# Strassen's scheme for the products with w1 and w2, with g and w34 kept in DRAM between two phases

## What is computed

```python
k_p = k.reshape(B, H, Sp, 8, D).mean(axis=3)            # 72 pooled keys per head, v_p likewise
scores = scale * q @ k_p.T;  attn = exp(scores - max);  attn /= attn.sum() + 1e-9
x = attn @ v_p                                          # 4608 x 512
a, b = x @ w1, x @ w2                                   # w1, w2: 512 x 1024
x = ((a * b) @ w3) @ w_out                              # w3: 1024 x 1024, w_out: 1024 x 512
logits = x @ w_gate + modality_bias[modality_id];  e = argmax(logits);  g = softmax(logits)[e]
out = g * (relu(x @ moe2_w1[e]) @ moe2_w2[e])           # one expert per token
```

## Time and profile before

| | |
|---|---|
| median of 3 runs | 1207.93 us |
| profiled execution | 1200.84 us |
| its span, first to last instruction | 1198.8 us |
| mean granted TensorE clock | 0.997 |

### The profile page before, as it was taken

The page is one execution under the profiler, slowest core; times in us unless marked ns, Lnnn a source line. Parts: engine busy times, 40 slices in busy tenths (PEclk is TensorE's granted clock), DMA queues, the critical chain, the costliest instruction groups (busy, mean ns, idle before and its releaser), DMA issues.

```text
span 1198.8 us, 26051 instructions
## 1 busy us (share of the span) xinstructions
PE 1181.9 (99%) x10830; PEld 1043.9 (87%) x10831; DVE 523.4 (44%) x1158; ACT 265.0 (22%) x517; POOL 210.9 (18%) x245
## 2 busy tenths in 40 slices
PE   9999999999999999999999999999999999999996
PEld 7888888989889788897888989898999999899895
DVE  1657556475563754746414144622222243222221
ACT  1233222222222222222212124111111141111110
POOL 2234222022220222102000001121221112121111
PEclk9999999999999999999999999999999999999998
DMA  9552132230231312303000005151111101111111
GB/s 350 175 190 85 70 104 85 72 119 36 87 102 52 103 63 86 111 30 94 10 28 1 36 1 202 34 183 58 44 61 35 44 26 54 44 45 51 35 50 39
DMA packets 43295, 92.76 MB, mean 77 GB/s; under 512 B 9411, under 2 KB 18755, under 8 KB 42180
## 3 DMA queue, kind: packets, MB, share of 16 engines
q1 hardware_dynamic: 34356, 66.68, 16.7%
q0 software_dynamic: 6400, 20.50, 5.3%
q10 hardware_dynamic: 2448, 4.26, 1.0%
HBM read 70.93 MB, written 21.01 MB: 77 GB/s over the span
## 4 chain that ended last, share of the span: by engine, by line
PE 96%; DVE 2%; DMA 1%; issue 0%; ACT 0%; POOLq 0%; DVEq 0%
PE ab L709 17%; PE ab L710 17%; PE ab L711 17%; PE rt L709 6%; PE x2p L709 6%; PE x2p L711 6%; PE x2p L710 6%; PE rt L710 6%; PE rt L711 6%; PE sct L780 3%; PE ab L802 2%; PE ab L728 2%; PE sct L878 1%; PE x2p L728 1%; DMA w3b<-in_moe_w 1%; PE rt L728 1%
## 5 line engine op out<-in xcount | busy, mean ns | idle before, releaser
L709 PE MATMUL ab<-xth,e1h 128*128 128x256 f32 x608 | 169.5, 279 | 1.5 <-issue 1.5
L710 PE MATMUL ab<-xtl,e1h 128*128 128x256 f32 x608 | 170.5, 280 | 0.0
L711 PE MATMUL ab<-xth,e1l 128*128 128x256 f32 x608 | 169.3, 278 | 0.0
L1152 ACT ACTIVATE hth<-ab 128x512 fp32r<-128x512 f32 x76 | 45.5, 598 | 341.8 <-PE ab L711 341.8
L1595 DVE SCALAR_TENSOR_TENSOR htl<-ab,hth 128x512 fp32r<-128x512 f32 x76 | 52.3, 691 | 157.1 <-ACT hth L1152 157.0
L709 PEld LDWEIGHTS ab<-xth,e1h 128*128 128x128 f32 x608 | 114.1, 188 | 2.6 <-issue 1.9
L709 PE MATMUL ab<-xh,w1h 128*128 128x512 f32 x288 | 116.1, 403 | 0.0
L1245 DVE TENSOR_TENSOR ac<-ab,ac 128x512 f32<-128x512 f32 x72 | 49.8, 691 | 149.6 <-PE ab L711 91.8
L710 PEld LDWEIGHTS ab<-xtl,e1h 128*128 128x128 f32 x608 | 114.4, 188 | 0.7
L711 PEld LDWEIGHTS ab<-xth,e1l 128*128 128x128 f32 x608 | 114.2, 188 | 0.0
L710 PE MATMUL ab<-xl,w1h 128*128 128x512 f32 x288 | 112.9, 392 | 0.0
(11 more groups left out here) (200 smaller groups left out, 2394.8 us busy)
## 6 DMA issues: line engine op xcount, KB each, us to landing
kv<-in_v SPq DMA_DIRECT2D x24, 512.0 KB, 4.8
qt<-in_q SPq DMA_DIRECT2D x8, 1280.0 KB, 6.3
kv<-in_k SPq DMA_DIRECT2D x16, 576.0 KB, 7.9
x_rows<-xr SPq DMA_DIRECT2D x36, 256.0 KB, 3.3
stage<-in_moe_w SPq DMA_DIRECT2D x8, 1024.0 KB, 9.7
vp<-v_rows SPq DMA_DIRECT2D x32, 192.0 KB, 3.7
w3b<-in_moe_w ACTq DMA_DIRECT2D x16, 256.0 KB, 5.5
wo_t<-in_w_out_t SPq DMA_DIRECT2D x4, 512.0 KB, 8.7
```

What stands on the lines that cost most here:

```text
L709: pe.matmul(outp, lh, rh, start=first, stop=False)
L710: pe.matmul(outp, lh, rl, start=False, stop=False)
L711: return pe.matmul(outp, ll, rh, start=False, stop=last)
L1152: act.activation(hth[:, 2 * n:2 * n + 2, :].rearrange("p f n -> p (f n)"), ab[n // 2][:, n % 2, :], ACT.Relu).then_inc(hth_ready, 1)
```

## The change

- **Order.** All nine stages of products with w1 and w2 run first, then all 36 groups of products with w34. g goes to DRAM (`g_rows`) and comes back group by group through five pairs of buffers (`RING`), and is split into hi and lo when it comes back. w34 goes to DRAM (`w34_rows`) from the start and comes back before the second phase. The leftover tokens of each batch go to DRAM too (`left_x`).
- **Strassen (Winograd's form).** For each of 4 positions in a stage, x (512 tokens by 512) and the weights are cut in 2 x 2 blocks; seven block products replace eight. The seven sums or blocks of x (`xf`: `x_sum`) and of w1, w2 (`wr`: `w_sums`) are formed and split ahead of them (`hi_x`, `lo_x`, `hi_w`, `lo_w`). Each `product` has 2 x 2 x 3 matmuls of 128x256 (w1 into one half of a bank, w2 into the other), and three banks are used in turn. DVE adds each product's bank onto partial sums (`kb`) in SBUF (seven additions of 128x512 per position, and one copy on ACT), then multiplies a by b (`g_first`, `g_rest`).
- **Softmax.** `soft_max` takes only the maxima and scales them; `exp_p` is eight activations of 128x72 per round, one for each head, straight from PSUM with the maximum as bias and the sum as a second output; `norm`, eight activations on ACT, replaces the multiplication on DVE. A new round of scores now waits for `exp_done` instead of `sub_done`. ACT issues the loads of q and the stores of g and w34.
- **Routing** tables run in the second phase, in banks that are free there.
- The expert stage is the same but for its places in SBUF.

The core of the diff ("..." for what is left out):

```diff
+BLOCKS = 7
+POS = FC // 2
+HT = MAIN // 2
+RING = 5
+TABLE_AT = {4: (0, 1), 6: (2, 3)}
...
+            def product(b, i, n):
+                at, fs = POS * b + i, slice(P * i, P * (i + 1))
+                bank = product_bank(at, n)
+                if i == 0:
+                    pe.wait_ge(xl_ready, BLOCKS * b + n + 1)
+                if n == 3:
+                    pe.wait_ge(x_copied, at + 1)
+                elif n > 3:
+                    pe.wait_ge(c_taken, 7 * at + n - 3)
+                elif at:
+                    pe.wait_ge(c_taken, 7 * at + n - 2)
...
+                for m in range(2):
+                    if b == 0 and i == 0:
+                        pe.wait_ge(wl_ready, BLOCKS * m + n + 1)
+                    for c in range(2):
+                        mm = split(bank[:, HT * m:HT * (m + 1)], wh[:, m, n, c, fs], wl[:, m, n, c, fs],
+                                   xh[:, n, c, :], xl[:, n, c, :], m == 0 and c == 0, m == 1 and c == 1)
+                mm.then_inc(prod_done[n], 1)
+
+            def position(b, i):
+                if i == 0 and b == 0:
+                    score(1, 0)
+                if i == 1 and b + 1 < B:
+                    score(b + 1, 2)
+                if i == 2 and b + 1 < B:
+                    score(b + 1, 4)
+                if i == 3 and b + 2 < B:
+                    score(b + 2, 0)
+                for n in range(BLOCKS):
+                    product(b, i, n)
+                    if i == 0 and n == 3 and b + 1 < B:
+                        score(b + 1, 1)
+                    if i == 1 and n == 3 and b + 1 < B:
+                        score(b + 1, 3)
+                    if i == 2 and n == 6 and b + 1 < B:
+                        weigh_v(b + 1, 0)
+                    if i == 3 and n == 2 and b + 1 < B:
+                        weigh_v(b + 1, 1)
...
             def exp_p(b, m):
-                act.wait_ge(sub_done, AT * b + m + 1)
-                act.activation(pb[:, :], pb[:, :], ACT.Exp, scale=D ** -0.5 / POOL).then_inc(exp_done, 1)
+                r = AT * b + m
+                act.wait_ge(max_taken, r + 1)
+                if r > 1:
+                    act.wait_ge(p_turned, r - 1)
+                for h in range(H):
+                    ins = act.activation(pb[r % 2][:, KEYS * h:KEYS * (h + 1)],
+                                         sct[:, h // PAIRS, KEYS * (h % PAIRS):KEYS * (h % PAIRS + 1)], ACT.Exp,
+                                         bias=nmx[r % 2][:, h:h + 1], scale=D ** -0.5 / POOL,
+                                         accum_out=sm[r % 2][:, h:h + 1])
+                ins.then_inc(exp_done, 1)
+                if r + 2 < AT * B:
+                    act.dma_start(qt[:, r % 2, :, :], q[r + 2]).then_inc(q_in[r % 2], 16)
...
+                if i == 1:
+                    copy_x(at)
+                    if att:
+                        norm(b + 1, 1)
+                    store_g(at - 1, 1)
+                    if att:
+                        exp_p(b + 1, 2)
+                    store_g(at, 0)
...
+                if i == 3:
+                    if att:
+                        raw_x(b + 1, 0, range(2))
+                    copy_x(at)
+                    if att:
+                        raw_x(b + 1, 0, range(2, 4))
+                    store_g(at - 1, 1)
+                    if b < B:
+                        hi_x(b + 1, 0)
+                    if b + 2 < B:
+                        exp_p(b + 2, 0)
+                    store_g(at, 0)
...
+            def chain(at, n, to, of, order):
+                dve.wait_ge(prod_done[n], at + 1)
...
+                dve.tensor_tensor(pair(kb[:, to, :, :]), product_bank(at, n), pair(kb[:, of, :, :]),
+                                  ALU.add).then_inc(c_taken, 1)
...
+            def group(b, g):
+                t = G * b + g
+                if t + 2 < NG:
+                    lo_g(t + 2)
+                if g:
+                    take_logits(b, g - 1)
...
+                elif b:
...
+                    if g == 2:
+                        for n in range(2):
+                            route_onehot(b - 1, n)
+                    if g == 3:
+                        for n in range(2, G):
+                            route_onehot(b - 1, n)
+                        route_add(b - 1)
```

More of the change, by code:

```diff
@@ L49 @@
 HB = 3
[L51 to L52 removed]
 W3_BUFS = 4
 LEFT = 4
[L55 removed]
+PIECE_AT = {4: 0, 5: 1, 6: 2, 7: 3}
 WARM = 40
```

1109 lines of the change are left out of this document (655 added, 454 removed).

## The result

The changed kernel takes 1282.26 us (median of 4 runs, 1280.12 to 1282.96), the kernel before 1208.22 beside it. The ratio is 1.0614, 95% interval 1.0592 to 1.0637. Forecast were 1260 us with 1215 to 1305 as the range, and slower with 0.90. The profiled execution took 1280.12 us, 79.3 more than that of before, where the sum in the prediction had 55.5 more.

A forecast was written before the change was run, and what follows sets the result against it. PE was taken to bound the kernel everywhere; 1200.84 - 38.5 + 69 + 6 + 1.5 + 15.5 + 2 = 1256.3 us, plus half of the 7.1 by which the runs' median lies higher, gave 1260 us, range 1215 to 1305.

The forecast's parts named there:

- fewer matmuls: Products: 1728 matmuls of 128x512 become 3024 of 128x256, 392.3 us become 353.8, a gain of 38.5 us.
- waits in the products: Products phase: PE waits for ACT and DVE, 9.5 us a middle stage, 69 us in all.
- start: Before the products: ACT has 42 us of work where PE has 37, four banks hide part; 6 us, bounds 2 and 14.
- tables and ranks in the second phase: Second phase: PE waits for routing tables behind DVE's split of g, 13.5 us, and for the last ranks, 2 us.
- The pace: All matmuls: time from start to start is their cost, 0.227 us for 128x512 and 0.117 for 128x256.
- The recorded durations as pace: Rival, products: matmuls cost their recorded 0.279 and 0.392 us, +166 us, 1365; chance 0.03 together with g coming back late.
- e: Softmax on ACT: price of a round of eight exponentials with sums, taken as 2.5 us, between 1.0 and 3.7.
- The stepping: Middle stage: the three engines' lists followed in order give 9.5 us of PE waits and a stage of 57 us.
- The slope: Products phase: about 30 us per us of exponential round; waits 32 us at the low end, 117 at the high.
- dear exponentials: Rival, products: a round of exponentials costs 3.1 us or more and delays scores and additions; 1280 to 1305, chance 0.24.
- Faster: Rival, products: banks and buffers absorb most counted waits, about 10 us stay in the phase; 1187, chance 0.05.
- The forecast as it stands: Whole kernel: a round of exponentials costs 1.6 to 3.1 us; 1235 to 1280, chance 0.45.

The follow-up runs named there:

- e7_pace: The changed kernel with only the experts' transposed rows (high and low half) at other SBUF addresses; ratio 1.0568.
- e13_place: The changed kernel with x and its low part 32 bytes further on and the experts' high part 512 bytes further on; ratio 1.0600.
- e5_noread: The changed kernel with the exponentials' second-output sums dropped and one reduction on DVE taking them instead; 1268.73 us, ratio 1.0531.
- e2_single: The changed kernel with one exponential and one normalising activation a round instead of eight each, part of the softmax left out; ratio 1.0324.
- e10_shared: The changed kernel with one maximum for all eight heads of a row, one exponential a round and sums on DVE; ratio 1.0452.
- e3_start: The changed kernel with ACT's and DVE's operations at the start in another order; ratio 1.0564.
- e12_best: The changed kernel with five edits: one-hot rows earlier, start reordered, one shared maximum, other addresses, sums of x between additions; 1223.06 us, ratio 1.0146.
- e1_onehot: The changed kernel with DVE making the one-hot rows before splitting the next group of g in the second phase; ratio 1.0503.
- e4_xfirst: The changed kernel with DVE making sums of x and low halves before finishing g in each stage's third position; ratio 1.0638.

## Why the prediction was right, and where not

By its own steps, with the parts of the span (1278.4 - 1198.8 = 79.6):

| step | forecast | measured |
|---|---|---|
| fewer matmuls | -38.5 | 3024 x 0.1197 - 392.3 = -30.3 |
| waits in the products | +69 | +54 (what the rest leaves of 50.2) |
| start | +6 (2 to 14) | +22.7 |
| between the phases | +1.5 | +1.0 |
| tables and ranks in the second phase | +15.5 (3 to 22) | +17.7 (15.8 and 1.9) |
| the first gather | +2 (0 to 6) | +7.6 (5.2, and 2.4 by the clock) |
| experts | 0 | +6.7 |

- **What bounds it** was right: the earlier trace rows left no wait that could hide another, and most of the loss is PE's new idle time. Two parts of it are not: the pace of the matmuls (8.2 and 5.5 us) and the clock (about 9).
- **The pace** was the right quantity, but 0.117 was taken as that of the form. It is 0.120 at the places that the change gives the operands (e7_pace and e13_place show it); 8.2 us of gain were missing in the products, and 5.5 of the experts' 6.7 are this. Of the prediction's signs, the 0.117 for `xh`, `wh` did not come. The recorded durations as pace (1365) are out, as the earlier trace rows said.
- **e** was taken as 2.5 us a round and measured 0.297 x 8 = 2.4. The parts of it weren't right: the activation costs 0.205 where I had 0.24, the sum 0.09 where I had 0.07. The Trainium skill (VectorE: DVE Perf Modes, section "The TRN2 errata — SBUF-src ops pay a fixed extra latency per instruction"), set aside in the prediction for the 0.12 of the earlier trace rows, gives 0.20 for an activation of 72 columns from PSUM; e5_noread agrees with it, at 0.205, and the earlier trace rows don't. `norm` was taken as 1.6 from the slope of the earlier trace rows and is 2.07, 0.25 for each; the same section's figure for SBUF, 224 + 72 cycles, is 0.247, and here too the trace agrees.
- **The stepping** gave 57 us for a middle stage, and they are 56.1 to 57.1, but by two errors that cancel. The recorded waits are shorter than stepped: the stage from 272.9 has 0.43 and 1.16 at the second and third product (forecast 0.7 and 1.5), 0.53 at the seventh (0.6), 0.37 and 0.83 at the scores (0.6 and 1.6), 1.7 at the weighing (2.4), 0.7 at the first scores (0.8), 0.5 at the addition behind `soft_sum` (1.3); 6.6 with a last one of 0.4, not 9.5. A recorded wait is less than what it costs, since the matmul ahead of it is recorded for 0.28 us and paces at 0.12, and the first matmul behind it takes 0.22: read from starts, these waits cost 8.1 us. The other error is in the rest of the stage, 48.9 us where the prediction has 47.6, for the pace (0.9) and for scores and weighing. One reason for the shorter waits is that a DMA issue does not hold ACT's running instruction, as I had it with 0.4 us each from the earlier trace rows: the issue at 306.12 lies beside exponentials that keep their 0.30.
- **The slope**, 30 us for each us of e, was wrong. e2_single took 1.5 us from e and 1.3 from `norm` and the products lost 24 us; e10_shared took 1.7 from e, gave DVE 0.7, and they lost 17. It is 8 to 10 us per us. The forecast for the low end, 32, is met by e2_single (54 - 24 = 30), though with a shorter `norm` than it assumed; the one for the high end, 117, would by this slope be far too high, which no run tested.
- **The start** is the term that failed, 6 against 22.7, outside its bounds. I compared ACT's total work with PE's, 42 with 37 us, and took four banks as cover; the order of the two lists, which I had stepped through for a middle stage, I did not step through here. It makes ACT and DVE wait for each other in every round: at least 7.5 us by e3_start, 9.3 by shorter rounds alone (e2_single), 12.3 with both in e12_best. The granted clock is the second part, which I had excluded because no gap would be much longer than 1.5 us: the gaps were 6.8, 5.7 and 5.2, the clock fell around all three, and it cost about 9 us.
- **The tables** were seen where they are, by the order on DVE, and e1_onehot removes them. A group lost 1.13 us instead of 1.0. The ranks cost 1.9, as forecast. The second phase lasted 239 us, not about 225: 7.6 are the gather with its clock, 2.2 the tables and ranks, and most of the rest are the tables' own matmuls and the first transposes, which the 225 left out.
- **The rivals**: *dear exponentials* gives the measured time (1280 to 1305) for a reason that isn't the one at work, since e was 2.4. *Faster* is out: phase waits are 54 us, not under 25. The forecast as it stands gave 1235 to 1280, and the median lies 2 us above that: the time is in the range because the range took in the dear rival, and that is luck as far as the number goes. That the change is slower, and by waits of PE for ACT and DVE, is not luck.

The sum was thus 24 us low: the start (17), the pace and the experts (15), the gather (6), the tables (2), less the waits in the products, which were put 15 too high.

## What to carry to other kernels

Saving an eighth of the matmuls pays only if the engines that make the operands and take the results have idle time at the right moments: here each product of 1.4 us brings an addition of 0.7 on VectorE, and every softmax step that stands ahead of it in the list costs PE time. Step through the lists of every stretch, the start too, and ask of each wait what is queued behind it on its own engine; where two engines' lists wait for each other, the total of their work says nothing. Put work whose inputs are ready into the idle time ahead of a wait (the one-hot rows, worth 16 us), and when an operation that you didn't touch becomes slower, look at the address of its operand.

## What the runs showed of the hardware that was not expected

- The pace of fp32r matmuls of 128x256 is 0.117 or 0.120 us depending on whether a moving operand begins at an odd multiple of 32 bytes or all at multiples of 64. At 260 columns the second phase has 0.120 too, in all kernels.
- An activation with a sum as second output is two instructions: the second is recorded at 0.2 us and adds 0.09 to the pace. One of 128x72 from PSUM with a bias column paces at 0.205, one in place with a scale column at (2.07 - 0.34) / 7 = 0.25.
- A matmul engine idle for 6.8 us found its clock at 0.57 of full for the next 7 us, with a part of w34 at 6.21 us instead of 3.77. In e4_xfirst the lower level also came behind a wait of 1.9 us between products, and some 97 matmuls of the products started 0.213 us apart instead of 0.120.
